# Dilated values loaded from GpSimd's queue, and key copies and the softmax addend on ScalarE

## The reference, cut to what matters

```python
scores = scale * np.matmul(q, k.transpose(0, 1, 3, 2))
mask_plain = (rel >= 0) & (rel < window)                               # window 32, heads 0 to 3
mask_dil = (rel >= 0) & (rel < window * dilation) & (rel % dilation == 0)   # dilation 4, heads 4 to 7
scores = np.where(masks[None, :, :, :], scores, -1000000000.0)
scores = scores - np.max(scores, axis=-1, keepdims=True)
attn = np.exp(scores)
attn = attn / (np.sum(attn, axis=-1, keepdims=True) + 1e-09)
return np.matmul(attn, v)
```

## Time and profile before

| | |
|---|---|
| median of 3 runs | 856.87 us (856.0 to 858.98) |
| the profiled execution, its own time | 854.68 us |
| its span, first to last instruction | 852.8 us |
| busy share: PE, DVE, ACT, POOL | 97%, 71%, 57%, 9% |

### The profile page before, as it was taken

One profiled execution on the slowest core, in us unless ns is written; L12 is line 12 of the kernel. 1 busy time (PEld: TensorE's weight loads), 2 busy tenths in 40 slices (PEclk: granted clock), 3 DMA queues, 4 the chain that ended last, 5 costly groups with the idle time before them and its releaser, 6 DMA issues.

```text
span 852.8 us, 15550 instructions
## 1 busy us (share of the span) xinstructions
PE 823.2 (97%) x5046; PEld 753.6 (88%) x5046; DVE 608.7 (71%) x1187; ACT 489.9 (57%) x948; POOL 75.7 (9%) x129
## 2 busy tenths in 40 slices
PE   7999999989999999999999999999999999999994
PEld 5778787879999999999989999989999998999993
DVE  7888887876555555555577777798777788777762
ACT  4567767644455454444466666676666676666652
POOL 3112112240100000000000000011000003000002
PEclk9999999999999999999999999999999999999998
DMA  7597886255535434434431211223121214122001
GB/s 148 121 223 180 192 192 197 64 151 170 185 124 162 148 123 125 148 128 144 124 100 52 73 63 62 73 89 111 51 75 50 75 49 149 55 70 67 9 1 74
DMA packets 114913, 93.79 MB, mean 110 GB/s; under 512 B 65816, under 2 KB 94488, under 8 KB 114848
## 3 DMA queue, kind: packets, MB, share of 16 engines
q1 hardware_dynamic: 109920, 78.81, 32.5%
q0 software_dynamic: 4928, 14.16, 5.0%
HBM read 83.51 MB, written 9.44 MB: 109 GB/s over the span
## 4 chain that ended last, share of the span: by engine, by line
PE 84%; DVE 6%; issue 3%; DMA 2%; ACT 2%; POOL 1%; another core or an unknown queue 0%; POOLq 0%; DVEq 0%; ACTq 0%; SPq 0%
PE bank L765 24%; PE bank L763 24%; PE bank L764 24%; PE bank L625 2%; PE bank L604 2%; DMA xtok<-x_rows 2%; PE bank L613 1%; PE bank L588 1%; DVE shifted L1271 1%; DVE row_max L1268 1%; PE bank L706 1%; ACT probs L947 1%; PE bank L805 1%; DMA x_rows<-osb 1%; DVE kT L334 1%
## 5 line engine op out<-in xcount | busy, mean ns | idle before, releaser
L763 PE MATMUL bank<-yh,up_l 128*128 128x384 f32 x384 | 129.4, 337 | 0.5 <-DVE yl L1619 0.5
L765 PE MATMUL bank<-yh,up_h 128*128 128x384 f32 x384 | 129.5, 337 | 0.0
L764 PE MATMUL bank<-yl,up_h 128*128 128x384 f32 x384 | 128.9, 336 | 0.0
L765 PE MATMUL bank<-dn_h,hid 128*128 128x512 f32 x288 | 113.9, 396 | 0.0
L763 PE MATMUL bank<-dn_h,hid 128*128 128x512 f32 x288 | 112.5, 391 | 1.4 <-DVE hid L1597 1.4
L764 PE MATMUL bank<-dn_l,hid 128*128 128x512 f32 x288 | 113.8, 395 | 0.0
L1344 DVE TENSOR_TENSOR dn_l<-dn_raw,dn_h 128x512 fp32r<-128x512 f32 (+1 forms) x79 | 71.8, 909 | 54.5 <-ACT dn_h L998 52.5
L1141 ACT ACTIVATE work<-bank 128x384 f32<-128x384 f32 x96 | 47.2, 492 | 79.7 <-PE bank L765 78.7
L998 ACT ACTIVATE dn_h<-dn_raw 128x512 fp32r<-128x512 f32 (+1 forms) x79 | 63.7, 806 | 41.8 <-PE bank L765 41.8
L1153 ACT ACTIVATE work<-work 128x384 f32<-128x384 f32 x96 | 50.5, 526 | 63.8 <-DVE work L1592 61.8
L763 PE MATMUL bank<-xh,up_l 128*128 128x352 f32 x256 | 83.9, 328 | 2.0 <-DVE XS L1479 1.0
(11 more groups left out here) (212 smaller groups left out, 1692.4 us busy)
## 6 DMA issues: line engine op xcount, KB each, us to landing
up_raw<-in_moe_w_dram SPq DMA_DIRECT2D x32, 512.0 KB, 3.6
dn_raw<-in_moe_w_dram SPq DMA_DIRECT2D x32, 512.0 KB, 3.6
up_raw<-in_moe_w_in_dram SPq DMA_DIRECT2D x24, 512.0 KB, 3.4
dn_raw<-in_moe_w_out_dram SPq DMA_DIRECT2D x24, 512.0 KB, 3.6
qn<-in_q_dram SPq DMA_DIRECT2D x32, 144.0 KB, 2.9
kn<-in_k_dram SPq DMA_DIRECT2D x32, 144.0 KB, 3.3
xtok<-x_rows SPq DMA_DIRECT2D x4, 1152.0 KB, 7.6
x_rows<-osb POOLq DMA_DIRECT2D x8, 288.0 KB, 3.5
```

What stands on the lines that cost most here:

```text
L763: mm(o, w[1], x[0], start=first, stop=False, skip_group_check=True)
L764: mm(o, w[0], x[1], start=False, stop=False, skip_group_check=True)
L765: return mm(o, w[0], x[0], start=False, stop=last, skip_group_check=True)
```

## The change

1. The 8 DMAs that load the values of a dilated pair go from SP's queue to POOL's (`load_dilated_v`). They are issued there right behind the store of the pair two places ahead of it (p - 2), under semaphores of their own (`dil_v_in`). SP's program keeps its order without them.
2. Of the four blocks of turned keys, ScalarE copies three: half 1 of head 0 is added behind the two that it had. VectorE copies one. TensorE waits for a third semaphore, `k_head`.
3. The addend 1e-9 (`denominators`) is put on by ScalarE for step s - 2, at the start of iteration s, ahead of `exps`. VectorE takes the reciprocal from it.

```diff
-        def half_out(copy, p, half, first=False):
+        def half_out(copy, p, half, first=False, heads=(0, 1), signal=None):
-            for h in range(2):
+            for h in heads:
...
-            last.then_inc(tr_out[half], 1)
+            last.then_inc(signal or tr_out[half], 1)
...   (SP)
-                    load_v(b, p)
+                    if p < PAIRS // 2:
+                        load_v(b, p)
                     if p == PAIRS - 1:
                         with sp.If(b > B - 2):
                             load_expert(0, 0, 0, 2)
...   (POOL)
+            def load_dilated_v(b, p):
+                slot = p % 2
+                pool.wait_ge(pv_done, b * STEPS + 3 * p + 3)
+                pool.sem_inc(carrier, 1)
+                for h in range(2):
+                    vr = v[bass.ds(b, 1), 2 * p + h].rearrange("o (i a r) d -> r i (o a) d", a=2, r=2)
+                    for t, j0, j1, r, i0 in V_PARTS:
+                        pool.dma_start(vw[slot][j0:j1, t:t + 4:3, h, 0:D], vr[r, i0:i0 + j1 - j0]).then_inc(dil_v_in[slot], 16)
...
                     if p < PAIRS // 2:
                         pool.dma_start(xb.rearrange("(t p) c -> p t c", p=QT), o).then_inc(stored[slot], 16)
+                        load_dilated_v(b, p + PAIRS // 2)
...   (TensorE)
                     for half in range(2):
                         pe.wait_ge(tr_out[half], b * 2 * PAIRS + 2 * p + 3)
+                    pe.wait_ge(k_head, b * PAIRS + p + 1)
...
-                    pe.wait_ge(v_in[p % 2], b * (PLAIN_IN + DIL_IN) + (PLAIN_IN if p < 2 else PLAIN_IN + DIL_IN))
+                    pe.wait_ge(v_in[p % 2] if p < 2 else dil_v_in[p % 2], (b + 1) * (PLAIN_IN if p < 2 else DIL_IN))
...   (ScalarE)
                 half_out(lambda o, x: A(o, x, ACT.Copy), p, 0, first)
+                act.wait_ge(tr_done, b * 4 * PAIRS + 4 * p + 12)
+                half_out(lambda o, x: A(o, x, ACT.Copy), p, 1, first, (0,), k_head)
+
+            def denominators(b, s):
+                act.wait_ge(pv_done, b * STEPS + (s + 7))
+                act.wait_ge(inv_done, b * STEPS + (s + 3))
+                s %= STEPS
+                A(denom[:, s % 2, :], bank[6 + s % 2][:QT, 0:4 * VN].rearrange("p (a c) -> p a c", a=4)[:, :, D],
+                  ACT.Copy, bias=1e-9).then_inc(denom_done, 1)
...
+                    if s >= 2:
+                        denominators(b, s - 2)
+                    else:
+                        before_this(act, b, lambda: denominators(b, s - 2))
                     exps(b, s)
...   (VectorE)
-                half_out(cp, p, 1, first)
+                half_out(cp, p, 1, first, (1,))
...
-                dve.wait_ge(pv_done, G(7))
-                ts(denom[:, s % 2, :], o[:, :, D], 1e-9, None, ALU.add).then_inc(denom_done, 1)
                 dve.wait_ge(denom_done, G(3))
                 V.reciprocal(inv[:, s % 2, :], denom[:, s % 2, :]).then_inc(inv_done, 1)
-                dve.wait_ge(inv_done, G(3))
+                dve.wait_ge(inv_done, G(5))
```

More of the change, by code:

```diff
@@ L199, in fused_kernel @@
         v_in = [sem(f"v_in{i}") for i in range(2)]
+        dil_v_in = [sem(f"dil_v_in{i}") for i in range(2)]
         tr_done = sem_from("tr_done", 8)
         tr_out = [sem_from(f"tr_out{i}", 1) for i in range(2)]
+        k_head = sem("k_head")
         init_v = sem("init_v")
@@ L210, in fused_kernel @@
         denom_done = sem_from("denom_done", 2)
-        inv_done = sem_from("inv_done", 2)
+        inv_done = sem_from("inv_done", 4)
         norm_done = sem_from("norm_done", 4)
@@ L366, in load_v @@
                     vb = v[bass.ds(b, 1), 2 * p + h]
[L367 to L378, removed]
+                    sp.dma_start(vw[slot][WINDOW:, 0, h, 0:D], vb[:, 0:QT].rearrange("o p d -> (o p) d")).then_inc(v_in[slot], 16)
+                    later_tiles = vb[:, QT - WINDOW:QT - WINDOW + (NT - 1) * QT].rearrange("o (t p) d -> p (o t) d", p=QT)
+                    sp.dma_start(vw[slot][0:QT, 1:NT, h, 0:D], later_tiles).then_inc(v_in[slot], 16)
+                    late = vb[:, QT:NT * QT].rearrange("o (t p) d -> p (o t) d", p=QT)[QT - WINDOW:]
+                    sp.dma_start(vw[slot][QT:P, 1:NT, h, 0:D], late).then_inc(v_in[slot], 16)
             def load_rows(b):
@@ L987, in _ @@
                         before_this(act, b, lambda: squares(b, SQUARE_STEPS.index(s)))
+            denominators(B, -2)
             probsT_out(B, -1)
+            denominators(B, -1)
             def weights_hi(w, which, raw, hi, i, J, per, slots_free, parts=1, part=0):
```

## The result

The changed kernel takes 865.83 us (median of 4 runs, 863.33 to 866.44) against 857.35 for the kernel before; the ratio is 1.0095, 95% interval 1.0077 to 1.0114: slower by 8.5 us. The profiled execution took 866.18 us, with a span of 864.6 against 852.8 us, so 11.8 us are to be found in the traces. It is one of the longer of its four runs, and the profiled execution of the kernel before, 854.68 us, is shorter than each of the four behind 857.35; so some 3 of the 11.8 us are not in the medians.

A forecast was written before the change was run, and what follows sets the result against it. Attention was taken as bound by a ring of waits through VectorE, ScalarE and PE, and by the `xtok` store-and-load chain. Terms -0.4 (ring), +0.2 (pair 3), +3.6 (weights) gave +3.4 us: 860.3 from 856.87, range 854.5 to 864.

The forecast's parts named there:

- +3.6 for the weights: Last batch: SP issues expert weights early, they hold POOL's transfers, and PE waits for pair 2's values: +3.6 us, once.
- The step that failed: Pair 2's values in second and third batch: landing 2.8 us after issue, in time for PE; 0, bound 0 to 0.5 each.
- The ring, -0.10 a pair: Loop of waits through VectorE, ScalarE and PE setting a pair's 7.83 us; fewer key copies on VectorE save 0.10 a pair.
- The rival that VectorE sets the ring and PE's idle is freed: Attention: the change frees PE's idle, 0.28 us a pair over 16 pairs, -4.5 us, 852.4; chance 0.10.
- The gain ahead of the first square goes into the wait for `xtok`: Three later batches: pairs 0 and 1 gain 0.2 us together, which goes into ScalarE's 0.93 us wait; no net gain.
- The addend, 0.2, the key block, 0.41, an issue, 0.67: Unit prices: ScalarE's addend 0.2 us, its key block 0.41 us, each issue of a values load on POOL 0.67 us.
- everything behind attention moves as a block: Stages after attention, the first 137 us: unchanged in length, so only attention's length was priced.
- Pair 3 of the first batch, +0.2: First batch: pair 3's values from POOL's queue land too late for PE, +0.2 us.
- the rival of fair turns: Last batch: POOL's queue gets half of 380 GB/s beside the weights, so values land in time; 856.7, no change; chance 0.24.
- POOL is late in every dilated pair: All 8 dilated pairs: issues of 0.86 us make values 1.1 to 1.5 late, 866 to 869 with the collision; chance 0.08.
- ScalarE is late: All 16 pairs: a 0.4 us addend or squares delay the exponential by 0.2 each, plus the collision, 863.5; chance 0.10.

The follow-up runs named there:

- e1: Kernel before with only the dilated values moved to POOL's queue; key copies and addend stay on VectorE; ratio 1.0102 to the kernel before.
- e12: e1, but the loop loads one of six tiles of `xtok`, the rest behind attention; no comparable ratio (tail changed), attention 128.76 us against 123.95 before.
- e3: Changed kernel with SP holding the first expert's weights until pair 2 of the last batch is normalised; ratio 1.0116 to the kernel before.
- e2: Kernel before with only the two ScalarE parts, third key block and addend; all loads stay on SP; ratio 1.0028 to the kernel before.
- e9: Kernel before with only the third block of turned keys moved to ScalarE; ratio 0.9983 to the kernel before.
- e10: Kernel before with only the denominators' addend moved to ScalarE; ratio 1.0005 to the kernel before.
- e6: Changed kernel with 20 useless products on PE in each batch after the first, where it had idled; ratio 1.0146 to the kernel before.
- the two halves: Kernel before with the queue part alone (e1, ratio 1.0102) and with the two ScalarE parts alone (e2, ratio 1.0028).
- e8: e1 with SP also waiting in pairs 2 and 3 until that pair's middle product is done; ratio 1.0047 to the kernel before.
- e4: Changed kernel with the loads of values issued on POOL ahead of the store instead of behind it; ratio 1.0085 to the kernel before.
- e11: Kernel before with both ScalarE parts, last probabilities copied ahead of last addends, later squares, and only pair 3's values on POOL; ratio 0.9994 to the kernel before.
- e14: Kernel before with 17 semaphore increments nobody waits for in POOL's loop, no load moved; ratio 0.9998 to the kernel before.

## Why the prediction was wrong

The direction was right, the size not: 3.4 us forecast, 8.5 measured, outside the range. The term that gave the direction, +3.6 for the weights, set nothing in the changed kernel, so that the direction came out is in part luck.

- **The step that failed** is "in the second and third batch only `xtok` is in the way ... 0, with 0 to 0.5 each as the bound". I took the landing of 2.8 us from the earlier trace rows, stores with nothing large beside them, for loads that go out while `xtok` moves. The earlier trace rows had the right kind of row, a store held to 6.1 us by `xtok`, and I used it for the weights alone. The values took 6.1 to 6.7 us. Nor had I read the landing of these very loads beside `xtok` on SP's queue, 4.6 to 5.7 us in the kernel before, which showed that only their head start had kept them in time. e1 shows the price, 1.9 and 1.8 us of PE's waiting, and e12 the cause, since both go with `xtok`. In the changed kernel the two batches took 2.75 and 4.09 us more.
- **The weights, +3.6 once.** The mechanism exists where nothing hides it: 3.76 us in e12. That the price agrees is partly chance, since my sum had all of `xtok` ahead of the weights and e12 has a sixth of it. In the changed kernel they set nothing (e3), because I left out that `xtok` itself would be late in the last batch. It is issued 0.54 us ahead of the row maximum of step 41 instead of 2.71; the pause of 1.67 us on POOL is the larger part of that. So the last batch lost 3.70 us by another wait; that this is close to the forecast is luck.
- **The ring, -0.10 a pair.** It gave 0.24. I had priced the earlier row maximum and not PE's 0.20 us of idle behind the early one, which falls away too, with 0.14 us behind the turn's start. The rival that VectorE sets the ring and PE's idle is freed, 0.28 a pair, was right in that. The first 19 steps gained 1.70, with a wait for pair 2's values in them; 0.95 of it lies in steps 2 and 5 alone.
- **The gain ahead of the first square goes into the wait for `xtok`:** right, in e2 and e9 (1.7 us where the earlier trace rows has 0.93).
- **The addend, 0.2, the key block, 0.41, an issue, 0.67:** 0.17, 0.40 and 0.64. That everything behind attention moves as a block left out the price of the addend: 0.8 to 0.9 us ahead of the first turn and 0.5 in the last stage (e10).
- **Pair 3 of the first batch, +0.2:** it waited for nothing. Pair 2 did there: PE stood 0.73 us ahead of its product, and step 9 took 0.98 more.
- **The clock** had no term. Three stretches at 1.2 GHz stand beside 2.7 us that the two halves don't explain. In e6, with the idle filled, they are gone, which fits the idle as their cause; but e1 idled as long without one, and what each costs is not shown.
- **Held or in turns.** The earlier trace rows and now e1 against e12, 5.5 to 6.2 against 2.4 to 3.0 us, show that a load on POOL's queue is held by a large one on SP's. SP's own small loads are held as well (4.6 to 5.7 us in the kernel before), so this is not the queue's doing alone. The Trainium skill, DMA: Bandwidth & Descriptors, section SWDGE vs HWDGE vs iDMA, has the engine take the two kinds of queue in turn; by that I had made the rival of fair turns, and these rows speak against reading it as an equal share.
- **The rivals.** "POOL is late in every dilated pair", 866 to 869, has the number nearest to the measured one, by a mechanism that did not come: its issues took 0.64 us, not 0.86, and pair 3's values were never waited for. "ScalarE is late" is not what was measured either: the ring got faster.

Not shown: which of `xtok`'s properties holds the values (its bytes or its many packets); why e1 costs more in time than in its trace, and e8 less; what POOL's pause is; why the third batch lost 1.8 us more than its two halves together.

## What to carry to other kernels

Price a moved transfer with a row in which the same neighbours move, not with a quiet one: a factor of two lay between them here. The old queue has such a row: read how long the same loads take there, and how far ahead of their use they go out. Before a load goes to another queue, list what large transfer runs at its hour in each batch; pair 3's loads had none in most batches and attention hardly noticed the move, pair 2's stood beside `xtok` in each batch but the first. And when an engine gets faster ahead of a fixed transfer, move what waits for the transfer too, or the gain is only more waiting.

## What the runs showed of the hardware that I had not expected

- POOL pauses 1.65 to 1.67 us, waiting for nothing that the profile shows, ahead of its 77th DMA in each kernel with all dilated values on its queue, wherever in time that DMA falls (in e4 it goes out at 113.2 us, in the changed kernel at 118.9). Kernels with fewer DMAs on it show none in attention.
- The end behind the last scatter has three lengths, 6.8 to 6.9, 9.5, and 9.7 to 9.9 us, the same to 0.2 us in all kernels with the same number of loads on POOL's queue.
- A wait of PE of 0.20 us cost 0.25 from the scores to the mask, more than half of it behind the wait.
- The granted clock halves for 3.4 us, or 6.8 (e3, e4, e11), beside an idle PE in the middle of a busy stage; one wait of 1.93 us in e1 did not bring it about, one of 1.75 in the changed kernel and one of 1.68 in e14 did.
- `xtok`'s load of 1.15 MB holds small loads on either queue: 4.6 to 5.7 us on SP's in the kernel before (2.4 to 2.7 without it), 5.5 to 6.2 on POOL's in e1 (2.4 to 3.0 in e12).
